# Top-k attention and an MLP on one core: nine transposes a duo over both tiles, paired value products, and a new order on GpSimd

## The reference, cut to what matters

```python
# q, k, v: [4, 8, 576, 64] float32
scores = scale * np.matmul(q, k.transpose(0, 1, 3, 2))      # 576 x 576 per head
kth = np.partition(scores, -32, axis=-1)[..., -32:-31]
scores = np.where(scores >= kth, scores, -1e9)               # the 32 largest of a row stay
scores = scores - np.max(scores, axis=-1, keepdims=True)
attn = np.exp(scores)
attn = attn / (np.sum(attn, axis=-1, keepdims=True) + 1e-09)
out = np.matmul(attn, v)                                     # [4, 8, 576, 64]
x = out.transpose(0, 2, 1, 3).reshape(2304, 512)
h = x @ w_in                                                 # [2304, 2048]
sp = np.where(h > 20, h, np.log1p(np.exp(np.minimum(h, 20))))
y = (h * np.tanh(sp)) @ w_out                                # [2304, 512]
```

## Time and profile before

| | |
|---|---|
| runs | 813.78 us median (812.22 to 815.32) |
| the profiled execution | 814.72 us, its span 812.9 us |
| TensorE clock granted, mean | 0.985 |
| PE busy | 746.2 us, 92% |
| VectorE busy | 701.9 us, 86% |
| ScalarE busy | 552.9 us, 68% |
| GpSimd busy | 550.4 us, 68% |
| the chain that ended last | PE 56%, GpSimd 23%, ScalarE 8%, VectorE 7% |

### The profile page before, as it was taken

How to read it: one execution, slowest core, us unless ns; L and a number is a source line. 1 busy time by engine, 2 the same in 40 slices (tenths; PEclk the granted TensorE clock), 3 DMA queues, 4 the chain that set the end, 5 groups by cost and what they waited for, 6 DMA issues and landing times.

```text
span 812.9 us, 16813 instructions
## 1 busy us (share of the span) xinstructions
PE 746.2 (92%) x6352; PEld 660.2 (81%) x6352; DVE 701.9 (86%) x1513; ACT 552.9 (68%) x994; POOL 550.4 (68%) x679
## 2 busy tenths in 40 slices
PE   3267879989999999989999999998999999999998
PEld 2156778877888888878888888888888888888896
DVE  5899999988899999889999999969999999996000
ACT  4567586774868686968586868685868686867320
POOL 4778658694767676777676767676676676768133
PEclk9999899998999999999999999999999999999999
DMA  8522000020110000111110000010110000000000
GB/s 275 206 60 59 8 8 15 25 65 7 51 37 21 8 21 11 48 36 35 37 35 8 21 8 25 20 47 8 50 37 22 7 21 8 18 1 14 2 14 26
DMA packets 27857, 28.87 MB, mean 36 GB/s; under 512 B 2432, under 2 KB 20864, under 8 KB 27264
## 3 DMA queue, kind: packets, MB, share of 16 engines
q1 hardware_dynamic: 27776, 27.80, 11.0%
HBM read 23.07 MB, written 4.72 MB: 34 GB/s over the span
## 4 chain that ended last, share of the span: by engine, by line
PE 56%; POOL 23%; ACT 8%; DVE 7%; issue 4%; DMA 2%; ACTq 0%; POOLq 0%
PE ps_y L347 18%; PE ps_u L334 18%; PE ps_s L295 7%; POOL p_sb L573 7%; PE ps_o L318 6%; PE ps_s L281 6%; POOL g_lo L559 5%; POOL p_sb L584 3%; DVE left L516 3%; DVE top L524 3%; ACT p_sb L416 2%; POOL g_hi L557 2%; POOL k_lo L537 2%; DMA q_raw<-q_in 1%; POOL w_lo L548 1%
## 5 line engine op out<-in xcount | busy, mean ns | idle before, releaser
L524 DVE MAX8 top<-left 128x8 f32<-128x576 f32 x432 | 303.8, 744 | 0.0
L334 PE MATMUL ps_u<-xT,win 128*128 128x128 f32 x2304 | 276.9, 279 | 1.9 <-ACT xT L433 1.9
L334 PEld LDWEIGHTS ps_u<-xT,win 128*128 128x128 f32 x2304 | 264.8, 193 | 12.6 <-issue 10.0
L573 POOL TENSOR_TENSOR p_sb<-x_sb,p_sb 128x576 f32<-128x576 f32 x144 | 201.7, 1423 | 79.4 <-ACT p_sb L408 79.4
L516 DVE MATCH_REPLACE8 left<-top,left 128x576 f32<-128x576 f32 x288 | 211.6, 742 | 0.0
L400 ACT ACTIVATE x_sb<-ps_s 128x576 f32<-128x576 f32 x144 | 85.8, 648 | 91.7 <-PE ps_s L281 91.5
L425 ACT ACTIVATE pT<-ps_s 128x640 f32<-128x640 f32 x144 | 93.3, 696 | 76.5 <-PE ps_s L295 76.4
L295 PE MATMUL ps_s<-ident,p_sb 128*128 128x128 f32 x720 | 97.8, 286 | 28.6 <-POOL p_sb L584 26.4
L347 PE MATMUL ps_y<-w_hi,g_hi 128*128 128x512 f32 x288 | 120.3, 418 | 0.7 <-ACT y_sb L456 0.7
L416 ACT ACTIVATE p_sb<-p_sb,neg_max 128x576 f32<-128x576 f32 x144 | 110.6, 773 | 8.0 <-POOL p_sb L573 7.8
L408 ACT ACTIVATE p_sb<-x_sb,limit 128x576 f32<-128x576 f32 x144 | 103.6, 773 | 18.2 <-POOL limit L564 18.2
(11 more groups left out here) (38 smaller groups left out, 714.3 us busy)
## 6 DMA issues: line engine op xcount, KB each, us to landing
k_raw<-k_in SPq DMA_DIRECT2D x16, 288.0 KB, 2.9
q_raw<-q_in SPq DMA_DIRECT2D x64, 64.0 KB, 1.9
v_sb<-v_in SPq DMA_DIRECT2D x16, 256.0 KB, 2.9
g_raw<-w_out SPq DMA_DIRECT2D x8, 512.0 KB, 3.9
win<-w_in SPq DMA_DIRECT2D x4, 1024.0 KB, 9.5
y_out<-y_sb SPq DMA_DIRECT2D x16, 256.0 KB, 2.0
q_raw<-q_in SPq DMA_DIRECT2D x8, 128.0 KB, 2.0
v_sb<-v_in SPq DMA_DIRECT2D x16, 32.0 KB, 2.8
```

Of the source, the lines that this page charges most:

```text
L334: mm = pe.matmul(ps_u[:, n % 2, i, :], win[:, k, P * f:P * f + P], xT[:, k, :], start=(k == 0), stop=(k == KC - 1), skip_group_check=True)
L524: dve.max(best[:, t, EIGHT * r + EIGHT:EIGHT * r + 2 * EIGHT], left[:, t, :]).then_inc(found, 1)
L573: pool.tensor_tensor(p, x_sb[:, s % XS, t, :], p, ALU.subtract).then_inc(arg_ready, 1)
```

## The change

- `transposes`: p of a duo is padded no more to 640 columns a tile. The two tiles lie side by side in `p_sb` (1152 columns, `KT` is now 9), and nine transposes of 128 columns take the place of two times five. The fifth holds the end of one tile and the beginning of the other. `pT_ready` is counted after the fourth and the ninth, and `copy_pT` copies 512 and 640 columns instead of 640 twice. The next scores wait for both copies before their first product.
- `values` still makes five products a head, over chunks 0 to 4 and 4 to 8 (`KV`, `SPLIT_AT`). v is laid out for that on the host: five chunks with zeros ahead of or behind the 576 rows, in three layouts for the three ways a pair is used, so a pair of buffers is loaded again each time the layout changes: 32 loads of 320 KB, contiguous for each partition, instead of 16 loads of 288 KB in two DMAs each. The zero fills of `v_sb` and `p_sb` go.
- `values` of duos 2i and 2i+1 both stand in the even slot 2i+4; `pT` is doubled for it. Odd slots have none.
- GpSimd's slot is now `negate(s-1)`, `split_g`, `split_w` (of the slot before), `normalise(s-2)`, `exponents(s-1)`, `split_q(s+3)`, `guard(s-1)`, `split_k`.
- `q_raw` has one buffer instead of two, and its load stands one duo later; `top` has two instead of four, and `topk(s)` waits for `negate(s-2)`.
- The order of the first loads: k0, q0, k1, w0, w1, q1, k2, k3, v0 to v3, q2, the four of `win`, and then q3 (before: k0, q0, k1, q1, v0, k2, q2, w0, k3, q3, v1 to v3, w1, the four of `win`, q4). ScalarE's `split_w` of chunks 1 to 6 stands one slot earlier.

```diff
-KT = 5
-WIDE = KT * P
-KEYS_LEFT = S - (KT - 1) * P
+KT = 2 * S // P
+KV = 5
+SPLIT_AT = 4
-XS, PS_, TS = 4, 3, 4
+XS, PS_, TS, LISTS = 4, 3, 4, 2
+def values_slot(s):
+    return (s | 1) + LAG_PT
+V_USES = [[] for _ in range(PPB)]
+for _s in range(DUOS):
+    for _t, (_g, _r, _c) in enumerate(tiles_of(_s)):
+        _w = 0 if _r is not None else 1 + _t
+        _uses = V_USES[_g % PPB]
+        if _r is None or _t == 0:
+            if _uses and _uses[-1][:2] == (_g, _w):
+                _uses[-1] = (_g, _w, _uses[-1][2], _s)
+            else:
+                _uses.append((_g, _w, _s, _s))
 def w_chunks_at(s):
-    return [c for c in range(WCHUNKS) if min(c, UP_SLOT) == s]
+    return [c for c in range(WCHUNKS) if max(c - 1, 0) == s]
...
             def load_q(s):
-                if s >= QS:
-                    sp.wait_ge(qlo_ready, s - QS + 1)
+                if s >= 1:
+                    sp.wait_ge(qlo_ready, s)
...
+            def load_v(pr, i):
+                g, layout, _, _ = V_USES[pr][i]
+                if i >= 1:
+                    sp.wait_ge(out_ready, V_USES[pr][i - 1][3] + 1)
+                sp.dma_start(v_sb[:, pr, :, :], v[g, layout, :, :].rearrange("p (k c) -> p k c", k=KV)
                              ).then_inc(v_loaded[pr], 16)
...
             load_k(1)
+            load_w(0)
+            load_w(1)
             load_q(1)
-            load_v(0)
             load_k(2)
+            load_k(3)
+            for pr in range(PPB):
+                load_v(pr, 0)
             load_q(2)
-            load_w(0)
-            load_k(3)
-            load_q(3)
-            for g in range(1, PPB):
-                load_v(g)
-            load_w(1)
             for k in range(KC):
                 sp.dma_start(win[:, k, :], w_in[P * k:P * k + P, :]).then_inc(win_loaded, 16)
             for s in range(DUOS + DOWN_SLOT):
-                if QS + 2 <= s + 4 < DUOS:
-                    load_q(s + 4)
+                if 3 <= s + 3 < DUOS:
+                    load_q(s + 3)
...
-                            if first and h == 0 and s >= LAG_PT + 2:
-                                pe.wait_ge(pT_copied, 2 * (s - LAG_PT - 2) + t + 1)
-                            elif first and h == 0 and s >= 1:
+                            if first and h == 0 and t == 0 and s >= LAG_PT + 2:
+                                pe.wait_ge(pT_copied, 2 * (s - LAG_PT - 2) + 2)
+                            elif first and h == 0 and 1 <= s < LAG_PT + 2:
                                 pe.wait_ge(x_copied, 2 * (s - 1) + t + 1)
...
                 pe.wait_ge(p_ready, 2 * s + 2)
-                for t in range(2):
-                    p = p_sb[:, s % PS_, t, :]
-                    flat = ps_s[:, t, :, :].rearrange("p h c -> p (h c)")
-                    for k in range(KT):
-                        mm = pe.transpose(flat[:, P * k:P * k + P], p[:, P * k:P * k + P], ident[:, :])
-                    mm.then_inc(pT_ready, 1)
+                flat = ps_s[:, :, :, :].rearrange("p t h c -> p (t h c)")
+                p = p_sb[:, s % PS_, :, :].rearrange("p t c -> p (t c)")
+                for k in range(KT):
+                    mm = pe.transpose(flat[:, P * k:P * k + P], p[:, P * k:P * k + P], ident[:, :])
+                    if k == SPLIT_AT - 1 or k == KT - 1:
+                        mm.then_inc(pT_ready, 1)
...
-                if s >= LAG_PT:
-                    values(s - LAG_PT)
+                for d in (s - LAG_PT - 1, s - LAG_PT):
+                    if d >= 0 and values_slot(d) == s:
+                        values(d)
...
             def copy_pT(s):
-                if s >= 1:
-                    act.wait_ge(out_ready, s)
-                for t in range(2):
-                    act.wait_ge(pT_ready, 2 * s + t + 1)
-                    flat = ps_s[:, t, :, :].rearrange("p h c -> p (h c)")
-                    act.activation(pT[:, t, :, :].rearrange("p k c -> p (k c)"), flat[:, 0:WIDE],
+                if s >= 2:
+                    act.wait_ge(out_ready, s - 1)
+                flat = ps_s[:, :, :, :].rearrange("p t h c -> p (t h c)")
+                for i, (a, b) in enumerate(((0, SPLIT_AT), (SPLIT_AT, KT))):
+                    act.wait_ge(pT_ready, 2 * s + i + 1)
+                    act.activation(pT[:, s % 2, a:b, :].rearrange("p k c -> p (k c)"), flat[:, P * a:P * b],
                                    ACT.Copy).then_inc(pT_copied, 1)
...
-                best = top[:, s % TS, :, :]
+                best = top[:, s % LISTS, :, :]
+                if s >= LISTS:
+                    dve.wait_ge(negmax_ready, s - LISTS + 1)
...
             for s in range(-2, DUOS + LAG_NORM):
-                if 0 <= s - LAG_NORM:
-                    guard(s - LAG_NORM)
                 if 0 <= s - LAG_EXP < DUOS:
                     negate(s - LAG_EXP)
                 m, j = divmod(s - MISH_SLOT - 1, GROUPS)
                 if m >= 0 and j < 2:
                     split_g(m, j)
+                for c in w_chunks_at(s - 1):
+                    split_w(c)
+                if 0 <= s - LAG_NORM:
+                    normalise(s - LAG_NORM)
                 if 0 <= s - LAG_EXP < DUOS:
                     exponents(s - LAG_EXP)
                 if s + 3 < DUOS:
                     split_q(s + 3)
-                if 0 <= s - LAG_NORM:
-                    normalise(s - LAG_NORM)
+                if 0 <= s - LAG_EXP < DUOS:
+                    guard(s - LAG_EXP)
                 if s > -2:
                     for g in splits_at(s):
                         split_k(g)
-                for c in w_chunks_at(s):
-                    split_w(c)
```

More of the change, by code:

```diff
@@ L134, in program @@
         k_loaded = [sem(f"k_loaded{i}") for i in range(RAWS)]
-        q_loaded = [sem(f"q_loaded{i}") for i in range(QS)]
+        q_loaded = sem("q_loaded")
         v_loaded = [sem(f"v_loaded{i}") for i in range(PPB)]
@@ L253, in _ @@
                         load_k(g + RAWS)
-                for g in range(PPB, PAIRS):
-                    if LAST_USE[g - PPB] + LAG_PT == s:
-                        load_v(g)
+                for pr in range(PPB):
+                    for i in range(1, len(V_USES[pr])):
+                        if values_slot(V_USES[pr][i - 1][3]) == s:
+                            load_v(pr, i)
                 m, j = divmod(s - DOWN_SLOT, GROUPS)
@@ L287, in transposes @@
             def transposes(s):
-                pe.wait_ge(x_copied, 2 * min(s + LAG_PT + 1, DUOS - 1) + 2)
-                pe.wait_ge(p_ready, 2 * s + 2)
-                for t in range(2):
-                    p = p_sb[:, s % PS_, t, :]
-                    flat = ps_s[:, t, :, :].rearrange("p h c -> p (h c)")
-                    for k in range(KT):
-                        mm = pe.transpose(flat[:, P * k:P * k + P], p[:, P * k:P * k + P], ident[:, :])
-                    mm.then_inc(pT_ready, 1)
+                if s + LAG_PT + 1 < DUOS:
+                    pe.wait_ge(x_copied, 2 * (s + LAG_PT + 1) + 2)
+                else:
+                    pe.wait_ge(x_copied, 2 * DUOS)
+                    pe.wait_ge(pT_copied, 2 * (s - 1) + 2)
+                pe.wait_ge(p_ready, 2 * s + 2)
+                flat = ps_s[:, :, :, :].rearrange("p t h c -> p (t h c)")
[4 more added lines that the diff above has]
+                        mm.then_inc(pT_ready, 1)
             def values(s):
                 m, j = divmod(s, PPB)
-                for g, _, _ in tiles_of(s):
-                    if s == FIRST_USE[g]:
-                        pe.wait_ge(v_loaded[g % PPB], 32 * (g // PPB) + 32)
+                for pr in range(PPB):
+                    for i, (_, _, first, _) in enumerate(V_USES[pr]):
+                        if first == s:
+                            pe.wait_ge(v_loaded[pr], 16 * i + 16)
                 if j == 0 and m >= 1:
@@ L308, in values @@
                         c = D * (j // 2)
-                        for k in range(KT):
+                        for k in range(KV):
                             for h in range(2):
@@ L312, in values @@
                                                v_sb[:, g % PPB, k, D * h:D * h + D],
-                                               pT[:, t, k, D * h:D * h + D],
-                                               start=(k == 0), stop=(k == KT - 1), skip_group_check=True)
+                                               pT[:, s % 2, SPLIT_AT * t + k, D * h:D * h + D],
+                                               start=(k == 0), stop=(k == KV - 1), skip_group_check=True)
                 else:
-                    for k in range(KT):
+                    for k in range(KV):
                         for h in range(2):
                             mm = pe.matmul(ps_o[D * h:D * h + D, j, :], v_sb[:, j, k, D * h:D * h + D],
-                                           pT[:, h, k, :],
-                                           start=(k == 0), stop=(k == KT - 1), skip_group_check=True)
```

(18 more changed lines are left out.)

37 lines of the change are left out of this document (12 added, 25 removed).

## The result

The changed kernel takes 792.17 us (median of 4 runs, 792.04 to 792.93) against 813.41 for the kernel before beside it: ratio 0.9739, 95% interval 0.9718 to 0.9759. The forecast was 794. The profiled execution took 792.04 us, its span 790.2.

What follows compares the result with a forecast made beforehand. PE was taken as the bound, with POOL right behind. Span 812.9 - 23.8 (slots 12 to 73) + 1.2 (start) + 1.2 (end) = 791.5, plus 1.8 outside = 793.3, said as 794 us; forecast band 788 to 800, range 786 to 806.

Steps and rivals of the forecast that it cites:

- main term: GpSimd's early normalise and guard; with transposes and pairs, slots 12 to 73 take 610.8 instead of 634.6 us, -23.8.
- the start: First loads and early slots up to PE's slot 12: +1.2 us, bounds 0 and +6.6.
- the end: Slot 74 has both last duos' values: +1.2 us.
- Transposes: PE's nine transposes instead of ten, 0.109 us each: 0.11 us saved a slot, 6.8 over 62 slots.
- Values in pairs: PE's even slot 10.96 us, odd 8.48, together 19.44, taken as 19.5 with seams; the products are the same.
- the early normalise takes back 3.2: At slot 12, normalise ahead of exponents cuts DVE's +4.4 us at the hand-over to PE to +1.2.
- both nearly full: After the change, PE at 9.75 us a slot and DVE at 9.71 a duo are both nearly full.
- v, the single q buffer, `top`: Reloads and waits from fewer buffers: 0 taken; bounds +4 us for v, 17 for `top` and q.
- Rival A: Only part comes: ACT sets the pace where k is split, GpSimd's order saves nothing there; 805 us, chance 0.17.
- C: Slower: POOL's loop through ACT takes some 10.8 us a slot, blocks 41.1; 842 us, chance 0.08.
- D: Odd slots' scores wait for the second pT copy, v's reload costs 4 us; 812 us, chance 0.05.
- B: More comes: the start costs PE nothing (1.2 us), pairs run without seams (1.9); 790 us, chance 0.10.

Runs made afterwards that it cites:

- e1: GpSimd's new order alone (guard at the slot's end ahead of split_k, normalise ahead of exponents) in the kernel before: 794.16 us, ratio 0.977.
- e6: The changed kernel with GpSimd's old order (guard first, normalise behind split_q): 814.14 us, 1.0028 to the kernel before.
- e2: The kernel before with only guard moved to the end of GpSimd's slot, ahead of split_k: 805.8 us, ratio 0.9911.
- e3: The kernel before with only normalise moved ahead of exponents: 800.88 us, ratio 0.9853.
- e4: The changed kernel with a tenth transpose, the ninth made twice: 797.49 us, 0.981 to the kernel before.
- e5: The changed kernel with the values of each duo in its own slot again: 796.01 us, 0.9808 to the kernel before.
- e7: The changed kernel with q1 behind w0 alone, q2 ahead of w1 and v, win's loads spread behind q4 to q7: 784.6 us.
- e8: As e7, with the first block's Mish behind copy_pT of slot 11 instead of ahead: 783.56 us, 0.9656 to the kernel before.

## Why the prediction was right, point by point

The mechanism of the main term was right. That the total came within 2 us is in part luck, since two misses nearly cancel. Slots 12 to 73 took 607.1 us, 3.7 less than the 610.8 forecast (1.6 of this in slots 12 to 17); the start took 2.6 more than forecast, and the end 0.2 less (50.0 us behind the start of slot 74 against 49.0 before).

- **The order on GpSimd** was the main term, and its mechanism held. Of the 23.8 us forecast from slot 12 on, of which transposes were 6.8, e1 shows 17.9 by the order. Slots 50 to 53 were forecast at 43.1 and took 43.1; slots 30 to 34 at 50.4 and took 50.9. e6 shows the other side: without it nothing is gained. What the prediction did not say is how the two halves divide; e2 and e3 do.
- **Transposes**: forecast 6.8 us (0.109 each) over slots 12 to 73, measured 5.2 by e4 and 5.5 by e5 against e1 (0.084 to 0.093 each). The prediction took the group's row alone; `down` behind nine transposes takes 0.02 us longer than behind ten (e4's rows), and this the row does not tell. The Trainium skill's figure ("TensorE: Matmul & The Clock Gate", Back-to-back issue gap: about 81 ns for a pair of 128 columns), which the prediction set beside it and did not take, is the nearer one.
- **Values in pairs**: forecast 19.5 us a pair of slots, measured 10.84 + 8.52 = 19.36. Forty products in a row take 2.33 us, not 2.48. Over 31 pairs, 19.36 instead of 19.5 is 4.3 us in the kernel's favour, with the dearer `down` already in it. The forecast gave pairing nothing, and e5 finds 3.8 for it.
- **The start** was the step that failed in size: forecast +1.2 us at slot 12, measured 133.10 - 129.25 = +3.85, and against what the order alone gives (e1, 126.6) it is +6.5. e7 takes 7.6 us off by the loads alone. DVE itself was forecast roughly: it started 0.9 us later, went on in duo 2 at 38.62 (forecast 40.2), and began duo 11 at 123.19, 2.8 us later than before (forecast 4.4). What failed is "the early normalise takes back 3.2". From DVE's start of duo 11 to PE's slot 12 all kernels with the old place of normalise take the same time, and all with the early one take longer, but for e8, which moves Mish out of copy_pT's way:

  | kernel | duo 11 on DVE | slot 12 on PE | between |
  |---|---|---|---|
  | before | 120.36 | 129.25 | 8.89 |
  | e2, guard alone | 115.45 | 124.34 | 8.89 |
  | e6, changed, GpSimd's old order | 123.56 | 132.43 | 8.87 |
  | changed | 123.19 | 133.10 | 9.91 |
  | e7, changed, other first loads | 115.57 | 125.12 | 9.55 |
  | e1, GpSimd's order alone | 116.04 | 126.63 | 10.59 |
  | e3, normalise alone | 120.49 | 131.45 | 10.96 |
  | e5, changed, values unpaired | 123.34 | 134.46 | 11.12 |
  | e4, changed, a tenth transpose | 123.19 | 133.73 | 10.54 |
  | e8, e7 and first Mish later | 115.57 | 122.86 | 7.29 |

  So in place of -3.2 GpSimd's new order costs 1.0 us there in the changed kernel (9.91 against 8.87 in e6). Where DVE is the bound, normalise waits for the reciprocal, exponents and exps come later, Mish behind them, and copy_pT stands behind Mish in ACT's queue. In slot 11 PE waited 4.78 us for it, and then `up` took 5.36 us at the lower clock instead of 3.8 (before the change the wait in this slot was 2.25 us, and `up` took 4.83); e1, e3 and e7 have the same wait of 4.77 or 4.78 us:

```profile
126.17 0.85 PE L298 MATMUL ps_s<-k_hi,q_hi 64*128 64x288 f32 x4 [4.78 <-ACT pT L448]
...
127.91 5.36 PE L357 MATMUL ps_u<-xT,win 128*128 128x128 f32 x32
```

  The prediction had seen this wait for slot 15 (2.6 us; it was 0.96) and not looked at slot 11, the first with a Mish before it.
- **What is late next**: "both nearly full" holds. PE's four slots are 38.72 us and DVE's four duos 38.82. From 345.9 to 511 us the chain of waits runs over DVE alone, and DVE's share of the chain grew from 7% to 31%. In that stretch the changed kernel's end follows topk, not PE, so a further saving on PE alone should give little there; no run here saves more on PE. In e4 and e5, whose PE blocks are 0.27 us longer or more, DVE's share is 9%: the two engines are that close.
- **v, the single q buffer, `top`**: taken at nothing, and found nearly so. `top` costs one wait of 0.6 us, and ACT waits for a q load only three times, all in the first 26 us. The two slots with reloads (20 and 22) take 11.00 and 10.99 us where a plain even one takes 10.85, and their mixed values alone are 2.48 against 2.33.
- Rival A fell by slots 50 to 53 (43.1, e1 43.5), C by blocks of 38.7, D by their scores without a wait. B had that pairs lose their seams, and had it small (1.9 us); its free start was wrong.

## What to carry to other kernels

When two engines are tied, a saving on one is worth little until the order on the other gives slack: here nine transposes, paired products and the new loads made the kernel 2 us slower alone (e6; the start has a part in that, but the plain stretches lost 2.3 us too), the reordered queue made it 18.6 us faster alone (e1), and both together 21.2. In an in-order queue put what releases another engine first (normalise) and a short instruction that waits for a third engine where its input is just ready and nothing long stands before it (guard). Then look at the start by itself: the order of the first loads cost 7.6 us (e7), as much as a third of the whole gain. Most of that mends what the change itself had spoilt: with the old loads e1 has DVE at duo 11 at 116.04, the changed kernel at 123.19, e7 at 115.57. Whether e7's order would also help the kernel before was not tried.

## What the runs showed that was not expected

- An added transpose of 128 columns costs 0.084 to 0.093 us in a stream, though its row says 279 ns and its group 0.11 a piece (e4).
- A table load of ScalarE starts as soon as the exps end and its Mish follows at once: in the changed kernel exps end at 121.64, the load is 1.28 us from 121.65, Mish starts at 122.95, 0.02 us behind the load's end.
- A wait of PE costs more than its length. In the windows around slot 11 of the changed kernel (columns as above) PE does nothing for 4.6 us, and the granted clock is 0.64 in the 6.9 us behind it, a mix of 1.2 and 2.4 GHz; `up` takes 5.36 us there instead of 3.8. e8 shortened this wait and met one of 2.78 us in slot 12, with 0.86 in the window of that slot, the third row from e8:

```profile
121.50:126.10 4.60, 0.00 (x0) 0.00 (x0) 4.60 (x11) 4.57 (x8) 2.60 (x5) 0.80 0.05 14
126.20:133.10 6.90, 6.90 (x44) 6.62 (x45) 6.90 (x15) 5.64 (x10) 5.98 (x6) 0.64 0.01 2
```
```profile
122.86:135.30 12.44, 12.44 (x105) 10.94 (x106) 12.44 (x27) 8.06 (x15) 10.88 (x12) 0.86 0.02 7
```
